# Second layer: the remainder of the activations moves from GpSimd to VectorE, one step late

## The reference

```python
def _moe2_ref(x, w_in, w_out):        # x 3072x384, w_in 384x2048, w_out 2048x384
    h = x @ w_in
    g = h * np.cos(h)
    return (g @ w_out).astype(np.float32)
```

## Time and profile before

| | |
|---|---|
| runs | 2314.4, 2314.76, 2317.61 us; median 2314.76 us |
| profiled execution | 2311.99 us, of which the span from first to last instruction 2310.2 us |
| PE busy over the span | 2217.6 us (96%), 15460 matmuls |
| DVE, ACT, POOL busy | 1005.3 us (44%), 744.4 us (32%), 689.5 us (30%) |
| granted clock of PE | 0.977 on average |
| second layer | from about 1898 us to the end |

### The profile page before, as it was taken

One profiled execution on the slowest core, in us unless ns is written; L12 is line 12 of the kernel. 1 busy time (PEld: TensorE's weight loads), 2 busy tenths in 40 slices (PEclk: granted clock), 3 DMA queues, 4 the chain that ended last, 5 costly groups with the idle time before them and its releaser, 6 DMA issues.

```text
span 2310.2 us, 40688 instructions
## 1 busy us (share of the span) xinstructions
PE 2217.6 (96%) x15460; PEld 1839.5 (80%) x15460; DVE 1005.3 (44%) x1621; ACT 744.4 (32%) x1288; POOL 689.5 (30%) x504
## 2 busy tenths in 40 slices
PE   3699998999999999999999999999999999999998
PEld 2688886788888888888888888888888877888887
DVE  4877752543222323232322322232323246777676
ACT  5555643211111111111111111111111126666665
POOL 3100001004533323232323233332323244444433
PEclk6689999999999999999999999999999999999999
DMA  5243332202111010111111111111111100000001
GB/s 159 65 125 98 100 88 90 86 22 58 41 28 32 27 46 28 31 30 29 31 41 32 27 32 27 43 29 32 28 31 27 45 23 14 14 14 14 0 14 68
DMA packets 85221, 102.35 MB, mean 44 GB/s; under 512 B 8384, under 2 KB 70144, under 8 KB 85120
## 3 DMA queue, kind: packets, MB, share of 16 engines
q1 hardware_dynamic: 85120, 100.91, 15.7%
HBM read 87.40 MB, written 8.75 MB: 42 GB/s over the span
## 4 chain that ended last, share of the span: by engine, by line
PE 74%; issue 12%; POOL 7%; DVE 5%; ACT 2%; SPq 1%; POOLq 0%; DMA 0%; DVEq 0%; ACTq 0%
PE p_h L597 5%; PE h L597 5%; PE h L599 5%; PE p_h L599 5%; PE p_h L598 5%; PE h L598 5%; POOL hlo L1104 5%; PE am_y L628 4%; PE am_y L627 4%; PE am_y L626 4%; PE chain_y L626 2%; PE chain_y L627 2%; PE chain_y L628 2%; PE o_y L626 2%; PE o_y L627 2%
## 5 line engine op out<-in xcount | busy, mean ns | idle before, releaser
L1083 POOL TENSOR_TENSOR acc<-acc,py 128x512 f32 (+1 forms) x252 | 325.1, 1319 | 743.1 <-DVE py L1387 743.1
L947 ACT ACTIVATE hhi<-h 128x512 fp32r<-128x512 f32 x182 | 109.0, 599 | 771.4 <-PE h L599 771.4
L1354 DVE SCALAR_TENSOR_TENSOR hlo<-h,hhi 128x512 fp32r<-128x512 f32 x182 | 125.9, 692 | 475.8 <-ACT hhi L947 475.8
L1354 DVE SCALAR_TENSOR_TENSOR hlo<-p_h,hhi 128x512 fp32r<-128x512 f32 x182 | 125.8, 691 | 406.0 <-ACT hhi L947 406.0
L1051 POOL TENSOR_TENSOR wlo<-stage,whi (+1 forms) x114 | 156.4, 1374 | 438.2 <-ACT whi L837 413.3
L597 PE MATMUL h<-xhi,whi 128*128 (+1 forms) x690 | 269.8, 391 | 2.9 <-DVE scr L1455 2.9
L597 PE MATMUL p_h<-xhi,whi 128*128 (+1 forms) x690 | 269.2, 390 | 0.1
L598 PE MATMUL h<-xlo,whi 128*128 (+1 forms) x690 | 269.1, 390 | 0.0
L599 PE MATMUL h<-xhi,wlo 128*128 (+1 forms) x690 | 268.9, 390 | 0.0
L599 PE MATMUL p_h<-xhi,wlo 128*128 (+1 forms) x690 | 268.5, 389 | 0.0
L598 PE MATMUL p_h<-xlo,whi 128*128 (+1 forms) x690 | 268.5, 389 | 0.0
(11 more groups left out here) (223 smaller groups left out, 4066.7 us busy)
## 6 DMA issues: line engine op xcount, KB each, us to landing
stage<-wcat SPq DMA_DIRECT2D x40, 768.0 KB, 4.3
pb<-p_scratch SPq DMA_DIRECT2D x84, 256.0 KB, 4.7
kq<-kqt SPq DMA_DIRECT2D x48, 192.0 KB, 3.4
kn<-krow SPq DMA_DIRECT2D x6, 768.0 KB, 5.1
kT<-kta SPq DMA_DIRECT2D x24, 192.0 KB, 4.8
v<-vrow SPq DMA_DIRECT2D x24, 192.0 KB, 4.7
kb<-krow SPq DMA_DIRECT2D x24, 192.0 KB, 5.0
out<-acc SPq DMA_DIRECT2D x6, 768.0 KB, 3.8
```

Source lines behind the costliest of these rows:

```text
L947: act.activation(hhi[:, j, :], hps[j % 2][:, 0:TILE], ACT.Relu).then_inc(s["hhi_done"], 1)
L1083: pool.tensor_tensor(y, y, py[:, d, :], ALU.add).then_inc(s["added"], 1)
L1354: dve.scalar_tensor_tensor(out=hlo[:, j, :], in0=hps[j % 2][:, 0:TILE], scalar=0.0, in1=hhi[:, j, :].bitcast(F32), op0=ALU.max, op1=ALU.su ...
```

## The change

POOL's loop of the second layer keeps only the two weight remainders of a turn, in the three passes that have them; the last pass has no work for POOL. DVE makes `hlo`: in every step, behind `r(s)` and ahead of the takes and of `g(s)`, it makes the remainder of the step before. The remainder of the last step stands behind the last `g`, ahead of the last three takes. The waits that PE and DVE have on `h2_split` are as they were.

```diff
     @block.gpsimd
...
-        for q in range(PASSES2):
+        for q in range(PASSES2 - 1):
             with pool.Fori(0, NT // 2) as tp:
-                for st in range(2 * CH):
-                    j = st % CH
-                    pool.wait_ge(s["hhi2_done"], (q * NT + tp * 2) * CH + st + 1)
-                    pool.tensor_tensor(hlo[:, j, :], gg[:, j % 2, :], hhi[:, j, :].bitcast(F32),
-                                       ALU.subtract).then_inc(s["h2_split"], 1)
-                    if q < PASSES2 - 1 and st in SPLITS:
-                        split_lo((q + 1) % 2, tp * 2 + SPLITS.index(st), PASSES1 + q + 1)
+                for st in SPLITS:
+                    split_lo((q + 1) % 2, tp * 2 + SPLITS.index(st), PASSES1 + q + 1)
...
     @block.vector
...
+        def split_h2(j, g):
+            dve.wait_ge(s["hhi2_done"], g + 1)
+            dve.tensor_tensor(hlo[:, j, :], gg[:, j % 2, :], hhi[:, j, :].bitcast(F32), ALU.subtract).then_inc(s["h2_split"], 1)
+
         def steps(q, tp, prev):
...
                 dve.scalar_tensor_tensor(out=r, in0=kint[:, j % 2, :], scalar=-C2, in1=r, op0=ALU.mult,
                                          op1=ALU.add).then_inc(s["r_done"], 1)
+                if prev or st > 0:
+
+                    split_h2((st - 1) % CH, g - 1)
                 if prev and 2 <= st < 5:
                     take(*prev, 1, st - 2)
...
             with dve.Fori(1, NT // 2) as tp:
                 steps(q, tp, (q, tp * 2 - 1))
+        split_h2(CH - 1, PASSES2 * NT * CH - 1)
         for t in range(DC):
             take(PASSES2 - 1, NT - 1, 1, t)
```

## The result

| | before | changed |
|---|---|---|
| median of 22 runs each | 2314.58 us | 2310.44 us |
| ratio, 95% interval | | 0.9975, 0.9967 to 0.9983 |
| profiled execution, span | 2310.2 us | 2305.1 us |
| POOL busy | 689.5 us | 537.0 us |

What follows compares the result with a forecast made beforehand. The prediction took PE's own matmul pace as the bound, so only its waits could be won: 4.2 + 1.3 + 0.3 = 5.8 us off the median of 2314.76 gives 2309.0 us, range 2306.8 to 2313.8.

Steps and rivals of the forecast that it cites:

- (a): Middle of the second layer: POOL loses 96 `hlo`, no r meets one, PE stops waiting; the whole 4.2 us go.
- (b): DVE gets 96 `hlo` at 684 ns each, hidden while it waits for |r| and cos; no wait of PE.
- (c): POOL's 18 weight remainders start earlier; r or the new `hlo` may lose 0 to 0.5 us, taken as 0.1.
- (d): After the first turn: PE starts 0.16 us earlier, later waits go; 1.3 us saved, bounds -0.8 to +1.5.
- (e): The layer's end: g 0.30 us later, last remainder 0.58 us shorter; 0.3 us saved.
- (f): The layer's start: PE waits for g of step 0, which holds no `hlo`; nothing changes.
- half of it: Small waits stay where step 7 has two takes; gain 2.9 us, 2311.9 us; chance 0.22 together with the clock.
- no gain: Middle waits come from takes and high parts, or are partly missing records; 2313.5 to 2315 us; chance 0.15.
- Slower: DVE's queue becomes the loop, `hlo` exposed in each step: 26 us slower, 2341 us; chance 0.08, 0.06 by the queue.
- The clock: PE's wait after the first turn ends with the lower clock, losing 1.5 us: 2310.5 us; chance 0.22 with half of it.
- what the prediction drew from it against the change: By the rule on shared SBUF interfaces, the new `hlo` on DVE can itself be held up; no size given.

Runs made afterwards that it cites:

- e1: Kernel before, with the second reduction r reading h from PSUM in place of r1 from SBUF; POOL still makes `hlo`: 2307.05 us, 0.9967 of before.
- e2: Changed kernel, with an idle two-operand subtraction on POOL in every step, when it used to make `hlo`: 2346.55 us, 1.0131 of before.
- e6: Changed kernel, with `hlo` moved behind g in DVE's queue: 2366.88 us, 1.0223 of before.
- e7: Changed kernel, with `hlo` moved behind the takes and ahead of g in DVE's queue: 2311.3 us, 0.9985 of before.
- e8: Changed kernel, with POOL's idle two-operand subtraction in every step started by `kint` instead of by the high part: 2321.01 us, 1.0027 of before.
- e3: Changed kernel, with an idle one-tile copy on POOL in every step, behind a one-column subtraction carrying the wait: 2311.17 us, 0.9974 of before.
- e4: Changed kernel, with the last two x tiles split in thirds inside the first turn instead of whole behind it: 2305.72 us, 0.9957 of before.
- e10: e4 plus `down` doing high-part products first, last two takes behind the last `hlo`, and first `up` and an x remainder moved earlier: 2304.38 us, 0.9944.

## Why the prediction was right

Step by step, from start to start of PE's matmuls:

| step | predicted | measured |
|---|---|---|
| (a) the middle | 4.2 us, all of it | 1555 starts in 352 us: all of it |
| (b) price of `hlo` on DVE | 684 ns, hidden | 685 ns, hidden |
| (c) weight remainders | 0.1 us on r | the 18 r beside them 0.69 us: nothing |
| (d) behind the first turn | 1.3 us | 3.7 to 2.4 us late in all: 1.3 |
| (e) the end | 0.3 us | 2.4 to 2.1 us late in all: 0.35 |
| (f) the start | 0 | 0.2 us, the low clock let go sooner |
| sum | 5.8 us | layer 6.3 us, times 5.8 us by the ratio |

(a) is right, and its reason holds in the main: e1 and e2 take the meeting of the two engines away or bring it back, and the time follows. The prediction left out that more than half of the late starts stood at `down`, for a `hlo` that the same meeting had stretched on POOL; the change takes that away as well, so the sum didn't suffer. In (c) the remainder ends 0.06 us behind the start of r and holds nothing up. The longest r, 0.81 us, is the first one (1903.03), beside POOL's last addition of the first layer. (b) rests on where `hlo` stands; e6 shows what another place costs (57 us; the reckoning with the same rows had given 60), and e7 that the slack at step 7 is what was worked out, to about 0.1 us. (d) had the right sum with one part off: the `x2_hi` of ACT came 1.3 us earlier against the layer's start, not 0.98, so DVE's `hlo` was ready earlier. (f) is chance, since it is the clock alone. In (e) g came 2.41 us behind r, for which 4 x 0.61 = 2.44 had been said.

Of the rivals, *half of it* and *no gain* did not come; the waits in the middle were real, no missing records. (By (d) and (e) alone *no gain* would have begun at 2314.76 - 1.6 = 2313.2 us, not at 2313.5.) *Slower* did not come either, but what it feared exists: e2 has the long `hlo`, e6 the work outside the shadow. *The clock* was not met behind the first turn in either profile of the changed kernel, and was in e6, e7 and e8. The contention that the Trainium skill names (GPSIMD Engine Reference, the row on SBUF interfaces) is what carries the case; the trace agrees for r and, in e2 and e3, for `hlo`. What the prediction drew from it against the change came to nothing, because just 18 weight remainders of POOL are left to meet, and they end as r begins.

Still open: how much of the 4.2 us was due to the held-up r and how much to POOL's stretched `hlo`. No run took away one without the other.

## What to carry to other kernels

Before moving an elementwise operation between GpSimd and VectorE, look for VectorE instructions with two operands in SBUF whose longest time is far over their shortest: what GpSimd does next to them may be on the path, though the hold-up itself is never named as a releaser: the waits of PE carry the name of the g or `hlo` that came late. A spread alone proves no cost, as e3 and the last pass of e8 show. Put the moved work where its new engine already waits, and work out the slack there from rows; the same 0.69 us of work costs nothing in one place and 57 us in all in another. And a loop that has time in hand again is worth more than the waits it saves: e4's gain is to be had only on top of the change.

## What the hardware showed that I had not expected

The two engines don't slow each other down, they go one after the other, and the one that started first isn't touched. In the kernel before, r begins first in 54 of the 96 steps and keeps 0.69 us, and POOL's `hlo` ends 1.15 us behind it. In the other 42 r ends 0.55 us behind the end of POOL's instruction, whether it began 0.04 us behind its start (r takes 1.79 us), 0.15 us (1.68) or 1.64 us (1.04). In e8 it is 0.55 us too, at distances of 0.5 to 1.0 us. So a few hundredths of a us decide whether POOL loses 0.4 us or DVE 1.0.

A plain copy on POOL, one operand, holds up a two-operand instruction of DVE (685 to 1034 ns in e3) and is held up by one, while DVE instructions with one operand in PSUM keep 0.68 us beside POOL's work in all of e2, e3 and e8.

The clock is a toss at a given wait. Behind the same wait for the first g (2.44 us idle, 2.32 in e1) the granted clock was at its lower level (1.2 GHz) in seven of twelve profiles and stayed at the upper one in five. A window of the changed kernel behind that wait, columns as in the earlier trace rows:

```profile
1906.12:1909.30 3.18, 3.18 (x8) 2.56 (x9) 2.29 (x4) 1.87 (x3) 0.00 (x0) 0.54 0.02 5
```

8 starts where 14 fit: 1.4 us. e7 fell behind a wait of 2.01 us after the first turn, and the changed kernel did not behind 2.17. So a profile can differ from another by 1.5 us per long wait for this alone, a quarter of what this change brings; e10, whose longest wait at the start is 0.54 us, kept the full clock there.
